# Seven half-depth products in place of eight for two chunks of a feed-forward layer's first product (TensorE, GpSimd)

## The chip, the cores and the metric

The kernel runs on one core of one Trainium2 chip. The metric is the device time of one execution in microseconds (us); the runs are given by their median.

## The reference, cut to what matters

An attention stage is followed by two feed-forward layers. The attention output `x` is taken as 1536 tokens by 512 features.

```python
def _moe_ref(x, w_in, w_out, a, b):        # first layer, d_ff = 2048
    h = x @ w_in
    ...
    return g @ w_out
def _moe2_ref(x, w_in, w_out):             # second layer, d_ff = 2048
    h = x @ w_in
    g = h - np.tanh(h)
    return g @ w_out
```

The change is in `h = x @ w_in` of the second layer: 1536x512 by 512x2048, in fp32.

## The kernel before, in words

Attention takes the first third of the time and is not touched. Each feed-forward layer is cut into three chunks of 512 tokens (`c`) and 16 weight tiles of 128 hidden units (`j`). One *step* `t` is one tile of one chunk; there are 48 steps in each layer, 96 in all (`NT`), and layer, chunk and tile of a step come from `place` (L758).

fp32 precision is had from three matmuls on rounded parts: every operand is kept as `hi` (rounded to fp32r) and `lo` (the rest), and hi*hi, hi*lo and lo*hi are summed in PSUM. So the first product of a step (`pe_g1`, L786) is 4 slices of depth x 3 terms = 12 matmuls of 128x512 into one of four PSUM banks `h_ps`, and the second (`pe_g2`, L811) is 4 blocks x 3 terms = 12 matmuls into the four banks `acc`, where the 16 tiles of a chunk are summed. TensorE's order is written out by hand (L1287): the first product of step t+4 (SKEW = 4), then the second of step t.

In the second layer a step asks of the other engines: ScalarE takes the tanh out of PSUM into `mag` (L880), VectorE subtracts it from `h_ps` into `pol` (L1019), ScalarE rounds that to `g_hi` (L857), which first waits until the second product of three steps earlier has freed one of the three buffers, and VectorE makes `g_lo` (L1025). In chunk 0, each step also splits one `w_in` and one `w_out` tile into hi and lo (L887 and L894 on ScalarE, L1033 and L1041 on VectorE); all 32 weight tiles stay in SBUF for the chunks 1 and 2. The layer's input of each chunk is copied out of `acc` (L911, `x2_raw`), rounded (L916) and its rest made (L1049), with the raw value and the rest in the same memory. The output leaves `acc` through VectorE's copies (L1060) and one store per 128 tokens on SP's queue (L1270 on). SP's queue loads the second layer's weights as the tiles of the first come free (L1267 on). GpSimd has no work in the feed-forward layers but for the splitting of 9 late tiles of the first (`pool_split_weights`, L763).

```python
for t in range(NT):                        # TensorE, L1287
    if t + SKEW < NT:
        pe_g1(eng, t + SKEW)
    pe_g2(eng, t)
```

Of the kernel before, what the change touches and what calls it, by code (L numbers as in the profile page):

```python
# [13 lines left out]
P = 128  # L14
# [16 lines left out]
def build(nc, q, k, v, proj, w_in1, w_out1, coef_a, coef_b, w_in2, w_out2,  # L31
# [42 lines left out]
            for names in ADDED_BY.values() for name in names}  # L74
    loads = {name: top.enter_context(nc.semaphore("s_" + name))
             for name in ["ident", "consts", "coefs", "ready", "coef", "proj", "q", "k", "v", "out", "ops0", "ops1",
# [7 lines left out]
                 "x2_raw", "x2_lo", "y", "early_hi", "early_lo", "low", "sum",  # L84
                 "last_norm", "last_hi", "last_lo"]}

# [4 lines left out]
    with top:  # L91
# [28 lines left out]
        g_lo = sb(top, "g_lo", [P, TEMPS, CH], F32R)  # L120

        def weight_slot(ctx, name):
            hi = sb(ctx, name + "_hi", [P, 512], F32R)
# [53 lines left out]
        for kind, j in LATE:  # L177
            (w_in_slot if kind == "in" else w_out_slot)[j] = weight_slot(mlp, f"w{kind}{j}")
        y_sb = [sqr[:, 0, :], sqr[:, 1, :], sqr[:, 2, :], mag[:, 2, :]]
        h_ps = [ps(mlp, f"h_ps{i}", [P, CH]) for i in range(4)]  # L180
        acc = [ps(mlp, f"acc{i}", [P, 512]) for i in range(4)]
# [589 lines left out]
        def pool_split_tiles(eng, numbers):  # L771
            for i in numbers:
# [3 lines left out]
                else:  # L776
                    pool_split_weights(eng, loads[f"w_out{j}"], w_out_slot[j], i)

        def split_in_count(layer, j):
# [31 lines left out]
        def pe_g2(eng, t):  # L811
            layer, c, j = place(t)
            _, w_hi, w_lo = w_out_slot[j]
            hi, lo = g_hi[:, t % TEMPS, :], g_lo[:, t % TEMPS, :]
            if c == 0:
                if layer == 0 and j < POOL_OUT:
                    eng.wait_ge(mlp_sems["early_lo"], POOL_TILES.index(("out", j)) + 1)
                else:
                    eng.wait_ge(mlp_sems["w_out_lo"], split_out_count(layer, j))
            eng.wait_ge(mlp_sems["g_lo"], t + 1)  # L820
            if t == 0:
                eng.wait_ge(sems["pt_lo"], BIAS + 2 * TILES * PAIRS)
                eng.wait_ge(mlp_sems["sum"], GROUPS)
            for i in range(4):
                cs = slice(i * P, (i + 1) * P)
                if j == 0 and t > 0:
                    if layer == 0 or c == 0:
                        eng.wait_ge(mlp_sems["x2_raw"], 4 * (t // J - 1) + i + 1)
                    else:
                        eng.wait_ge(mlp_sems["y"], 4 * (c - 1) + i + 1)  # L830
                if layer == 0:
                    terms = ((w_lo[:, cs], hi), (w_hi[:, cs], hi), (w_hi[:, cs], lo))
                else:
                    terms = ((hi[:, cs], w_lo[:, :]), (hi[:, cs], w_hi[:, :]), (lo[:, cs], w_hi[:, :]))
                for n, (l, r) in enumerate(terms):
                    mm = eng.matmul(acc[i][:, :], l, r if layer else r[:, :], start=j + n == 0,  # L836
                                    stop=j == J - 1 and n == 2)
                if j == J - 1 and i < 3:
                    mm.then_inc(mlp_sems["acc"], 1)
            mm.then_inc(mlp_sems["g2"], 1)  # L840


        def act_inverse_ln(eng, t):
# [4 lines left out]
        def act_inverse_exp(eng, t):  # L848
            eng.wait_ge(mlp_sems["ln"], t + 1)
            eng.activation(mag[:, t % TEMPS, :], mag[:, t % TEMPS, :], ACT.Exp, scale=-1.0  # L850
                           ).then_inc(mlp_sems["r0"], 1)

        def act_g_hi(eng, t):
            eng.wait_ge(mlp_sems["g"], t + 1)
            if t >= TEMPS:
                eng.wait_ge(mlp_sems["g2"], t - TEMPS + 1)
            eng.activation(g_hi[:, t % TEMPS, :], pol[:, t % TEMPS, :], ACT.Copy  # L857
                           ).then_inc(mlp_sems["g_hi"], 1)

        def act_reads(eng, t):  # L860
            b, hp = t % TEMPS, h_ps[t % 4][:, :]
            if place(t)[0] == 0:
                if t == 0:
                    for e in range(2):
                        eng.wait_ge(loads[f"ops{e}"], 128 * PAIRS)
                    eng.wait_ge(sems["lo"], BIAS + 2 * PAIRS)
                eng.wait_ge(mlp_sems["h"], t + 1)
                if t >= TEMPS:
                    eng.wait_ge(mlp_sems["g_lo"], t - TEMPS + 1)
                eng.activation(pol[:, b, :], hp, ACT.Identity, scale=ca[:, 3:4], bias=ca[:, 2:3])  # L870
                if t >= TEMPS:
                    eng.wait_ge(mlp_sems["g"], t - TEMPS + 1)
                eng.activation(mag[:, b, :], hp, ACT.Abs, scale=cb[:, 0:1])
                eng.activation(sqr[:, b, :], hp, ACT.Square).then_inc(mlp_sems["square"], 1)
            else:
                eng.wait_ge(mlp_sems["h"], t + 1)
                eng.wait_ge(mlp_sems["g"], t - 1)
                if t >= NT - J + SKEW:
                    eng.wait_ge(mlp_sems["y"], 4 * (NCH - 1))
                eng.activation(mag[:, t % 2, :], hp, ACT.Tanh).then_inc(mlp_sems["tanh"], 1)  # L880
# [38 lines left out]
        def act_x2(eng, t):  # L919
            c, step = x2_step(t)  # L920
            if 0 <= c < NCH and step == 0:
                act_x2_raw(eng, c)
            if 0 <= c < NCH and 1 <= step <= 4:
                act_x2_hi(eng, c, step - 1)

        def act_step(eng, t, reads=True):
# [14 lines left out]
            else:  # L941
                if t == L:
                    act_inverse_ln(eng, t - 1)
                    act_g_hi(eng, t - 2)
                    act_inverse_exp(eng, t - 1)
                if t < NT:
                    act_reads(eng, t)
                act_g_hi(eng, t - 1)
                act_x2(eng, t)
                if t < NT:  # L950
                    act_split_in(eng, t)
                    act_split_out(eng, t)


# [67 lines left out]
        def dve_g_lo(eng, t):  # L1022
            b = t % TEMPS
            eng.wait_ge(mlp_sems["g_hi"], t + 1)
            eng.tensor_tensor(g_lo[:, b, :], pol[:, b, :], g_hi[:, b, :].bitcast(F32),  # L1025
                              ALU.subtract).then_inc(mlp_sems["g_lo"], 1)
# [17 lines left out]
        def dve_x2(eng, t):  # L1044
            c, step = x2_step(t)
            if 0 <= c < NCH and 1 <= step <= 4:
                i = step - 1
# [4 lines left out]

        def dve_y(eng, c):
            for i in range(4):
                acc_ready(eng, NCH + c, i)
                if c == 0 and i == 0:
                    eng.wait_ge(mlp_sems["g"], TILES_LAYER)
                if c > 0:
                    eng.wait_ge(loads["out"], 64 * c)
                eng.tensor_copy(y_sb[i], acc[i][:, :]).then_inc(mlp_sems["y"], 1)  # L1060

        def dve_step(eng, t):
# [15 lines left out]
            else:  # L1078
                if t == L:
                    dve_g_lo(eng, t - 2)  # L1080
                    dve_inverse_times(eng, t - 1)
                    dve_g_neg(eng, t - 1)
                if t < NT:
                    dve_g_minus(eng, t)
                dve_g_lo(eng, t - 1)
                dve_x2(eng, t)
                if t < NT:
                    dve_split_in(eng, t)
                    dve_split_out(eng, t)
            if t % J == SKEW - 1 and t >= L + J:  # L1090
                dve_y(eng, (t - L) // J - 1)

        with nc.Block() as block:

            @block.sync
            def _(eng):
# [88 lines left out]
                def load_weight(layer, kind, j):  # L1185
# [7 lines left out]
                    else:  # L1193
                        if layer == 1:
# [3 lines left out]
                                      ).then_inc(loads[f"w_out{j}"], 16)  # L1198

                def sync_att(p, turn=True):  # L1200
                    if turn:
# [68 lines left out]
                for c in range(NCH):  # L1270
                    for i in range(4):
                        block = 4 * c + i
                        eng.wait_ge(mlp_sems["y"], block + 1)
                        eng.dma_start(out_d[:, block // T, block % T, :], y_sb[i]
                                      ).then_inc(loads["out"], 16)
                eng.wait_ge(loads["out"], 64 * NCH)

            @block.tensor
            def _(eng):
# [6 lines left out]
                pe_att(eng, PAIRS - 1, prepare=False, turn=False, last=True)  # L1286
                for t in range(NT):  # L1287
                    if t + SKEW < NT:
                        pe_g1(eng, t + SKEW)
                    pe_g2(eng, t)  # L1290

            @block.scalar
            def _(eng):
# [10 lines left out]
                act_att(eng, PAIRS - 1, prepare=False, turn=False, last=True)  # L1304
                for t in range(2, NT + 1):
                    act_step(eng, t)

            @block.vector
            def _(eng):
# [65 lines left out]
```

## Time and profile before

| | |
|---|---|
| median of 3 runs | 766.28 us (766.01 to 767.57) |
| the profiled execution, its own time | 768.19 us |
| its span, first to last instruction | 766.4 us |
| TensorE busy | 753.4 us, 98% of the span, 3840 matmuls |
| VectorE, ScalarE, GpSimd busy | 536.4, 478.0, 160.6 us |
| mean granted TensorE clock | 0.996 |

The span starts at the first instruction. A matmul's end is modelled, and matmuls are pipelined, so neighbours overlap in the rows; the distance of two starts tells what one costs. PE is TensorE's matmul side, PEld its weight loads, DVE VectorE, ACT ScalarE, POOL GpSimd, and a q behind a name (SPq) the engine's queue of instructions.

### The profile page before, as it was taken

The numbers are of one execution on the slowest core, as the hardware profiler recorded it, in microseconds if no ns is written. First come the engines' busy times: TensorE is split into PE (matmuls) and PEld (weight loads), VectorE is DVE, ScalarE is ACT, GpSimd is POOL, SyncE is SP. The second block draws the span as 40 slices with busy tenths as digits, with TensorE's granted clock in tenths as the row PEclk, the third lists the DMA queues.
The fourth block names the chain that finished last, engine by engine and source line by source line (L and its number), as shares of the span: only waits on it lengthen the run. The fifth ranks groups of instructions, "written<-read, shape, count | busy, mean of one in ns | idle before, by whom it ended". The sixth has DMA issues, their size and how long they took to land.

```text
span 766.4 us, 11961 instructions
## 1 busy us (share of the span) xinstructions
PE 753.4 (98%) x3840; PEld 644.6 (84%) x3840; DVE 536.4 (70%) x854; ACT 478.0 (62%) x938; POOL 160.6 (21%) x137
## 2 busy tenths in 40 slices
PE   5999999999999999999999999999999999999998
PEld 3999999999998788778888888888888888888886
DVE  4888888888997999999988898955542322233222
ACT  4989889888897778788767776755432222222221
POOL 5774574565579000000000000000000000000000
PEclk8999999999999999999999999999999999999999
DMA  7579778777655500000000123230000100001001
GB/s 196 128 173 211 171 171 199 177 178 180 163 128 154 183 1 1 0 1 1 0 1 15 55 86 107 88 91 1 0 1 1 56 0 1 0 1 56 0 1 56
DMA packets 65243, 58.11 MB, mean 76 GB/s; under 512 B 31792, under 2 KB 50480, under 8 KB 65200
## 3 DMA queue, kind: packets, MB, share of 16 engines
q1 hardware_dynamic: 63488, 57.09, 29.6%
q10 hardware_dynamic: 1712, 0.46, 0.3%
q8 instruction: 25, 0.41, 0.2%
q14 instruction: 18, 0.15, 0.1%
HBM read 29.57 MB, written 3.19 MB: 43 GB/s over the span
## 4 chain that ended last, share of the span: by engine, by line
PE 84%; DVE 12%; issue 2%; ACT 1%; ACTq 0%
PE acc L836 28%; PE h_ps L807 27%; PE slot L256 9%; PE turn_ps L382 8%; PE pv_ps L340 4%; PE pv_ps L342 4%; DVE pol L1001 2%; DVE sqr L980 2%; DVE pol L1012 2%; DVE pol L987 1%; DVE pol L993 1%; PE aux_ps L269 1%; DVE sqr L1004 1%; DVE g_lo L1025 1%; DVE wout_lo L1041 1%
## 5 line engine op out<-in xcount | busy, mean ns | idle before, releaser
L807 PE MATMUL h_ps<-x_hi,win_lo 128*128 128x512 f32 x384 | 149.7, 390 | 0.0
L807 PE MATMUL h_ps<-x_lo,win_hi 128*128 128x512 f32 x384 | 149.4, 389 | 0.0
L807 PE MATMUL h_ps<-x_hi,win_hi 128*128 128x512 f32 x384 | 149.4, 389 | 0.0
L857 ACT ACTIVATE g_hi<-pol 128x512 fp32r<-128x512 f32 x96 | 60.8, 634 | 126.0 <-PE acc L836 100.4
L1025 DVE TENSOR_TENSOR g_lo<-pol,g_hi 128x512 fp32r<-128x512 f32 x96 | 66.0, 687 | 97.9 <-ACT g_hi L857 97.7
L623 DVE TENSOR_TENSOR pt_lo<-turn_ps,pt_hi 128x384 fp32r<-128x384 f32 x192 | 97.8, 551 | 20.8 <-ACT pt_hi L530 20.0
L530 ACT ACTIVATE pt_hi<-turn_ps 128x384 fp32r<-128x384 f32 x192 | 85.0, 493 | 21.4 <-PE turn_ps L382 20.8
L581 DVE TENSOR_REDUCE row_min<-slot 128x1 f32<-128x768 f32 x96 | 90.8, 946 | 3.2 <-PE slot L256 2.8
L462 ACT ACTIVATE E<-slot,row_min 128x768 f32<-128x768 f32 x96 | 87.5, 911 | 1.9 <-issue 1.3
L807 PEld LDWEIGHTS h_ps<-x_lo,win_hi 128*128 128x128 f32 x384 | 72.2, 188 | 15.1
L807 PEld LDWEIGHTS h_ps<-x_hi,win_hi 128*128 128x128 f32 x384 | 72.1, 188 | 14.9
L807 PEld LDWEIGHTS h_ps<-x_hi,win_lo 128*128 128x128 f32 x384 | 72.1, 188 | 14.7
L382 PE MATMUL turn_ps<-ident,E 128*128 128x128 f32 x576 | 80.8, 275 | 0.0
L1019 DVE TENSOR_TENSOR pol<-h_ps,mag 128x512 f32<-128x512 f32 x48 | 33.2, 691 | 67.7 <-ACT mag L880 67.2
L880 ACT ACTIVATE mag<-h_ps 128x512 f32<-128x512 f32 x48 | 28.7, 598 | 78.4 <-PE h_ps L807 75.2
L836 PE MATMUL acc<-g_hi,wout_lo 128*128 128x512 f32 x192 | 75.0, 391 | 1.6 <-ACT x_raw L911 0.7
L836 PE MATMUL acc<-g_lo,wout_hi 128*128 128x512 f32 x192 | 74.7, 389 | 0.0
L836 PE MATMUL acc<-g_hi,wout_hi 128*128 128x512 f32 x192 | 74.7, 389 | 0.0
L836 PE MATMUL acc<-wout_lo,g_hi 128*128 128x512 f32 x192 | 74.7, 389 | 0.0
L836 PE MATMUL acc<-wout_hi,g_hi 128*128 128x512 f32 x192 | 74.7, 389 | 0.0
L836 PE MATMUL acc<-wout_hi,g_lo 128*128 128x512 f32 x192 | 74.7, 389 | 0.0
L382 PEld LDWEIGHTS turn_ps<-ident,E 128*128 128x128 f32 x576 | 68.1, 141 | 6.1 <-DVE pt_lo L623 0.6
(119 smaller groups left out, 1383.9 us busy)
## 6 DMA issues: line engine op xcount, KB each, us to landing
win_raw<-in_moe_w_in SPq DMA_DIRECT2D x32, 256.0 KB, 3.3
wout_raw<-in_moe_w_out SPq DMA_DIRECT2D x32, 256.0 KB, 3.0
q_nat<-in_q SPq DMA_DIRECT2D x16, 192.0 KB, 3.3
v_nat<-in_v SPq DMA_DIRECT2D x8, 384.0 KB, 3.3
k_nat<-in_k SPq DMA_DIRECT2D x14, 192.0 KB, 3.5
qA<-q_hi SPq DMA_DIRECT2D x14, 192.0 KB, 2.5
qB<-q_hi SPq DMA_DIRECT2D x14, 192.0 KB, 2.9
qB<-q_lo SPq DMA_DIRECT2D x14, 192.0 KB, 3.2
```

Source lines behind the costliest of these rows:

```text
L256: mm = eng.matmul(slot[m % 2][:, h, 0:HALF], ops[e][0][:, i * P:(i + 1) * P], ops[e][1][:, h * HALF:(h + 1) * HALF], start=first, stop=not ...
L340: eng.matmul(pv_ps[:, 0:HALF], vv, pt_hi[:, c % 2, kt, :], start=kt == 0, stop=False)
L382: mm = eng.transpose(turn_ps[h][:, c3 * P:(c3 + 1) * P], E[:, n % RING, kt * P:(kt + 1) * P], ident[:, :])
L462: eng.activation(halves(E[:, m % RING, :]), slot[m % 2][:, :, 0:HALF], ACT.Exp, bias=row_min[:, m % RING:m % RING + 1], scale=-1.0, accum_ ...
L530: eng.activation(pt_hi[:, c % 2, k0:k0 + T // 2, i * P:(i + 1) * P], turn_ps[h][:, 0:HALF].rearrange("r (k n) -> r k n", n=P), ACT.Copy).t ...
L581: eng.tensor_reduce(row_min[:, m % RING:m % RING + 1], slot[m % 2][:, :, 0:HALF], AX.XY, ALU.min).then_inc(sems["rowmin"], 1)
L623: eng.tensor_tensor(pt_lo[dst], turn_ps[h][:, 0:HALF].rearrange("r (k n) -> r k n", n=P), pt_hi[dst].bitcast(F32), ALU.subtract).then_inc( ...
L807: mm = eng.matmul(h_ps[t % 4][:, :], w[:, ws], columns(x, kt, c), start=kt + n == 0, stop=kt == KT - 1 and n == 2)
L836: mm = eng.matmul(acc[i][:, :], l, r if layer else r[:, :], start=j + n == 0, stop=j == J - 1 and n == 2)
L857: eng.activation(g_hi[:, t % TEMPS, :], pol[:, t % TEMPS, :], ACT.Copy).then_inc(mlp_sems["g_hi"], 1)
L1019: eng.tensor_tensor(pol[:, t % TEMPS, :], h_ps[t % 4][:, :], mag[:, t % 2, :], ALU.subtract).then_inc(mlp_sems["g"], 1)
L1025: eng.tensor_tensor(g_lo[:, b, :], pol[:, b, :], g_hi[:, b, :].bitcast(F32), ALU.subtract).then_inc(mlp_sems["g_lo"], 1)
```

## The change

For the chunks 1 and 2 of the second layer, the input and two weight tiles are taken as 2x2 blocks (two halves of depth by two chunks, and two halves of depth by two tiles). The four results come from seven half-depth products of 6 matmuls each, where before there were four full ones of 12 (eight halves). It is Winograd's form of Strassen's scheme. TensorE's work of the steps 0 to 59 stays as it is; `PLAIN` = 64 is the first step of chunk 1.

- The sums of input blocks (T1 to T4) are made once by VectorE in the steps 53 to 56 (`dve_sums`, 8 instructions), then the seven blocks are split in the steps 56 to 62 (14 roundings on ScalarE, 14 differences on VectorE). The 16 roundings and differences of chunks 1 and 2's own input (8 on each engine) fall away. T2, T3 and T4 take `w_out` slots 0 to 5.
- The sums of weight blocks (S1 to S4) are made once for each pair of tiles by GpSimd (`pool_s`): 10 sums of 128x256, then two roundings and two differences of 128x512. There are two buffers for them: `w_out` slots 6 and 7, and columns of chunk 0's input.
- TensorE (`pe_pair`) does for each of the 8 pairs the seven products, with second products in between: in pair 0 those of steps 60 to 63, one behind each of the products 0 to 3, in each later pair two of chunk 1, one behind product 3 and one behind product 6. Both second products of chunk 1 of pair 7 and the 16 of chunk 2 follow at the end.
- For each pair VectorE does 7 additions out of PSUM, 4 differences h - tanh(h) and 2 `g_lo` (`dve_pair`); ScalarE one copy out of PSUM, 4 tanh and 2 `g_hi` (`act_pair`). The values g of chunk 2 are kept in the `w_in` slots of the even tiles, which the pair has used.
- The eight overwritten `w_out` tiles are loaded and split again (`AGAIN`), one per pair (two in pair 1), into columns of chunk 0's input and the `w_in` slots of the odd tiles. The output of chunk 0 is copied in pair 0, three blocks in the middle, and the fourth, whose buffer waits for the first three stores, at its end.

```diff
+        PER_PAIR = 7
+        NPAIR = J // 2
+        BLOCKS = ["X11", "X21", "T2", "T3", "T1", "T4", "X22"]
+        WEIGHTS = ["W11", "W12", "S2", "S3", "S1", "W22", "S4"]
+        TAKEN = ["p1", "c11", "u2", "u3", "u4", "c21", "c12"]
+        RAW_STEP = PLAIN - 11
+        SPLIT_STEP = PLAIN - 8
+        S_OPS = 14
+        u_sum, u_more = pol[:, 2, :], mag[:, 2, :]
+        AGAIN = [0, 1, 7, 6, 5, 4, 3, 2]
+        AGAIN_STEP = [0, 1, 1, 2, 3, 4, 5, 6]
+        def bank(u, k):
+            return h_ps[(PER_PAIR * u + k) % 4][:, :]
+        def pe_product(eng, u, k):
+            if u == 0 and k < 4:
+                eng.wait_ge(mlp_sems["g"], PLAIN - 3 + k)
+            else:
+                eng.wait_ge(mlp_sems[TAKEN[(k - 4) % PER_PAIR]], u + (k >= 4))
+            if u == 0:
+                eng.wait_ge(mlp_sems["t_lo"], 2 * (k + 1))
+            if k in (2, 3):
+                eng.wait_ge(mlp_sems["s_ops"], S_OPS * u + 8 + 2 * k)
+            for kt in range(2):
+                w_hi, w_lo = w_block(u, WEIGHTS[k], kt)
+                _, b_hi, b_lo = x_block(BLOCKS[k], kt)
+                for n, (w, x) in enumerate(((w_lo, b_hi), (w_hi, b_hi), (w_hi, b_lo))):
+                    mm = eng.matmul(bank(u, k), w, x, start=kt + n == 0, stop=kt + n == 3)
+            mm.then_inc(mlp_sems["prod"], 1)
+        def pe_pair(eng, u):
+            t = PLAIN + 2 * (u - 1)
+            for k in range(PER_PAIR):
+                pe_product(eng, u, k)
+                if u == 0 and k < 4:
+                    pe_g2(eng, PLAIN - 4 + k)
+                if u > 0 and k == 3:
+                    pe_g2(eng, t)
+            if u > 0:
+                pe_g2(eng, t + 1)
...
+        def pool_s(eng, u):
...
+            eng.wait_ge(mlp_sems["w_in_lo"], split_in_count(1, pair_tile(u) + 1))
+            if u == 0:
+                eng.wait_ge(mlp_sems["g2"], TILES_LAYER + S_SLOT + 2)
+            elif u == 1:
+                eng.wait_ge(mlp_sems["h"], PLAIN)
+            else:
+                eng.wait_ge(mlp_sems["prod"], PER_PAIR * (u - 1))
+            sum_(a[:, one], h2[:, one].bitcast(F32), h2[:, two], ALU.add)
+            sum_(b[:, one], h1[:, one].bitcast(F32), h2[:, one], ALU.subtract)
+            sum_(a[:, one], a[:, one], l2[:, one], ALU.add, 1)
+            sum_(b[:, one], b[:, one], l1[:, one], ALU.add, 2)
+            sum_(a[:, one], a[:, one], l2[:, two], ALU.add, 3)
+            sum_(b[:, one], b[:, one], l2[:, one], ALU.subtract, 4)
+            sum_(a[:, two], a[:, one], h1[:, one], ALU.subtract, 5)
+            sum_(a[:, two], a[:, two], l1[:, one], ALU.subtract, 7)
+            sum_(b[:, two], h1[:, two].bitcast(F32), a[:, two], ALU.subtract, 8)
+            sum_(b[:, two], b[:, two], l1[:, two], ALU.add, 9)
+            for i, (raw, hi, lo) in enumerate(((a, a_hi, a_lo), (b, b_hi, b_lo))):
+                eng.wait_ge(mlp_sems["s_ops"], n + 10)
+                eng.tensor_copy(hi, raw).then_inc(mlp_sems["s_ops"], 1)
+                eng.wait_ge(mlp_sems["s_ops"], n + 11 + 2 * i)
+                eng.tensor_tensor(lo, raw, hi.bitcast(F32), ALU.subtract).then_inc(mlp_sems["s_ops"], 1)
...
+        def dve_pair(eng, u):
+            t, n = PLAIN + 2 * u, PER_PAIR * u
...
+            def add(k, out, other, signal):
+                eng.wait_ge(mlp_sems["prod"], n + k + 1)
+                eng.tensor_tensor(out, bank(u, k), other, ALU.add).then_inc(mlp_sems[signal], 1)
+            def minus_tanh(k, out, h, signal):
+                eng.wait_ge(mlp_sems["tanh2"], 4 * u + k + 1)
+                eng.tensor_tensor(out, h, mag[:, k % 2, :], ALU.subtract).then_inc(mlp_sems[signal], 1)
...
+            add(1, first, u_sum, "c11")
+            add(2, u_sum, u_sum, "u2")
+            add(3, second, u_sum, "u3")
+            add(4, u_more, second, "c22")
+            add(4, u_sum, u_sum, "u4")
+            if u == 0:
+                dve_y(eng, 0, range(3))
+            minus_tanh(0, first, first, "g")
+            add(5, second, second, "c21")
+            minus_tanh(1, kept_g(tile + 1), u_more, "kept")
+            dve_g_lo(eng, t)
+            add(6, u_sum, u_sum, "c12")
+            minus_tanh(2, second, second, "g")
+            minus_tanh(3, kept_g(tile), u_sum, "kept")
+            dve_g_lo(eng, t + 1)
+            if u == 0:
+                dve_y(eng, 0, range(3, 4))
...
-                for t in range(NT):
-                    if t + SKEW < NT:
-                        pe_g1(eng, t + SKEW)
+                for t in range(PLAIN - SKEW):
+                    pe_g1(eng, t + SKEW)
+                    pe_g2(eng, t)
+                for u in range(NPAIR):
+                    pe_pair(eng, u)
+                for t in range(NT - J - 2, NT):
                     pe_g2(eng, t)
```

## Rows read from the trace of the kernel before

**Rows 1.** The page: span, busy time of each engine, 40 slices of the span.
```profile
span 766.4 us, 11961 instructions
PE 753.4 (98%) x3840; PEld 644.6 (84%) x3840; DVE 536.4 (70%) x854; ACT 478.0 (62%) x938; POOL 160.6 (21%) x137
...
PEclk8999999999999999999999999999999999999999
```

**Rows 2.** The chain that ended last, in order of time: start us, us, what.
```profile
344.30 2.72 PE h_ps L807 x12
347.02 2.72 PE acc L836 x12
...
749.58 13.61 PE acc L836 x60
```

**Rows 3.** Windows, second layer: us, then busy (xcount) of PE, PEld, DVE, ACT, POOL.
```profile
680.00:760.00 80.00, 80.00 (x354) 66.26 (x354) 21.98 (x33) 17.25 (x28) 0.00 (x0) 1.00 0.04 14
```

**Rows 4.** Groups of DVE and ACT from 330 us on: busy us, mean ns | idle.
```profile
L1025 DVE TENSOR_TENSOR g_lo<-pol,g_hi 128x512 fp32r<-128x512 f32 x81 | 55.7, 688 | 97.9 <-ACT g_hi L857 97.7
L1019 DVE TENSOR_TENSOR pol<-h_ps,mag 128x512 f32<-128x512 f32 x48 | 33.2, 691 | 67.7 <-ACT mag L880 67.2
...
L1060 DVE COPY sqr<-acc 128x512 f32<-128x512 f32 x9 | 5.8, 685 | 4.7 <-PE acc L836 4.7
L857 ACT ACTIVATE g_hi<-pol 128x512 fp32r<-128x512 f32 x81 | 51.3, 634 | 112.3 <-PE acc L836 100.4 <-DVE pol L1012 10.9 <-DVE pol L1019 1.0
L880 ACT ACTIVATE mag<-h_ps 128x512 f32<-128x512 f32 x48 | 28.7, 598 | 78.4 <-PE h_ps L807 75.2 <-DVE mag L1060 3.2
```

**Rows 5.** Groups of POOL over the whole span, shapes apart.
```profile
L687 POOL TENSOR_TENSOR v_hl<-v_nat,v_hl 128x384 fp32r<-128x384 f32 x16 | 16.2, 1010 | 1.3
...
L653 POOL TENSOR_TENSOR k_lo<-k_t,k_hi 128x768 fp32r<-128x768 f32 x7 | 12.9, 1840 | 0.6
...
L768 POOL TENSOR_TENSOR wout_lo<-wout_raw,wout_hi 128x512 fp32r<-128x512 f32 x6 | 7.7, 1287 | 0.5
```

**Rows 6.** Timeline of POOL, 240 to 249 us: start us, us, what.
```profile
240.07 0.61 POOL L766 CAST wout_hi<-wout_raw 128x512 fp32r<-128x512 f32 x1
...
243.93 1.08 POOL L766 CAST wout_hi<-wout_raw 128x512 fp32r<-128x512 f32 x1
245.09 1.29 POOL L768 TENSOR_TENSOR wout_lo<-wout_raw,wout_hi 128x512 fp32r<-128x512 f32 x1
246.32 1.08 POOL L766 CAST win_hi<-win_raw 128x512 fp32r<-128x512 f32 x1
247.48 1.62 POOL L768 TENSOR_TENSOR win_lo<-win_raw,win_hi 128x512 fp32r<-128x512 f32 x1
```

**Rows 7.** Timeline of DVE over the same stretch.
```profile
243.48 1.06 DVE L980 SCALAR_TENSOR_TENSOR sqr<-sqr,cb_abs,mag 128x512 f32<-128x512 f32 x1
...
245.18 0.75 DVE L993 SCALAR_TENSOR_TENSOR pol<-pol,ca,h_ps 128x512 f32<-128x512 f32 x1
245.84 1.09 DVE L1001 SCALAR_TENSOR_TENSOR pol<-pol,ca,mag 128x512 f32<-128x512 f32 x1
246.86 1.09 DVE L1004 SCALAR_TENSOR_TENSOR sqr<-sqr,q_one,mag 128x512 f32<-128x512 f32 x1
247.99 1.67 DVE L1012 SCALAR_TENSOR_TENSOR pol<-sqr,pol 128x512 f32<-128x512 f32 x1
```

**Rows 8.** Timeline around 536 us, in the second layer's chunk 0.
```profile
535.46 0.69 DVE L1025 TENSOR_TENSOR g_lo<-pol,g_hi 128x512 fp32r<-128x512 f32 x1 [2.12 <-ACT g_hi L857]
...
536.07 0.68 DVE L1049 TENSOR_TENSOR x_lo<-x_raw,x_hi 128x512 fp32r<-128x512 f32 x1
...
537.03 0.39 PE L807 MATMUL h_ps<-x_lo,win_hi 128*128 128x512 f32 x1
...
537.45 0.60 ACT L880 ACTIVATE mag<-h_ps 128x512 f32<-128x512 f32 x1 [0.46 <-PE h_ps L807]
```

**Rows 9.** DMA issues: xcount, KB each, median us to landing.
```profile
wout_raw<-in_moe_w_out SPq DMA_DIRECT2D x32, 256.0 KB, 3.0
...
out<-sqr SPq DMA_DIRECT2D x9, 256.0 KB, 2.1
```

More of the change, by code:

```diff
@@ L84, in build @@
                  "x2_raw", "x2_lo", "y", "early_hi", "early_lo", "low", "sum",
-                 "last_norm", "last_hi", "last_lo"]}
+                 "last_norm", "last_hi", "last_lo",
+                 "t_raw", "t_hi", "t_lo", "s_ops", "prod", "p1", "u2", "u3", "u4", "c11", "c22", "c21", "c12",
+                 "tanh2", "kept"]}
     def begin(eng, who):
@@ L812, in pe_g2 @@
             layer, c, j = place(t)
-            _, w_hi, w_lo = w_out_slot[j]
+            if t >= PLAIN:
+                j = kept_tile(t)
+            _, w_hi, w_lo = again_slot[j] if t >= PLAIN and j in again_slot else w_out_slot[j]
+            first, last = t % J == 0, t % J == J - 1
             hi, lo = g_hi[:, t % TEMPS, :], g_lo[:, t % TEMPS, :]
@@ L825, in pe_g2 @@
                 cs = slice(i * P, (i + 1) * P)
-                if j == 0 and t > 0:
+                if first and t > 0:
                     if layer == 0 or c == 0:
@@ L835, in pe_g2 @@
                 for n, (l, r) in enumerate(terms):
-                    mm = eng.matmul(acc[i][:, :], l, r if layer else r[:, :], start=j + n == 0,
-                                    stop=j == J - 1 and n == 2)
-                if j == J - 1 and i < 3:
+                    mm = eng.matmul(acc[i][:, :], l, r if layer else r[:, :], start=first and n == 0,
+                                    stop=last and n == 2)
+                if last and i < 3:
                     mm.then_inc(mlp_sems["acc"], 1)
@@ new lines, in s_buffer, with w_block @@
+        def s_buffer(u):
+            if u % 2 == 0:
+                return [[part[:, :] for part in w_out_slot[S_SLOT + i]] for i in range(2)]
+            return [[columns(part, i, 0) for part in (x2_raw, x_hi, x_lo)] for i in range(2)]
+        def w_block(u, name, kt):
+            half = lambda t, i: t[:, (2 * i + kt) * P:(2 * i + kt + 1) * P]
+            if name[0] == "S":
+                n = int(name[1]) - 1
+                _, hi, lo = s_buffer(u)[n // 2]
+                return half(hi, n % 2), half(lo, n % 2)
+            _, hi, lo = w_in_slot[pair_tile(u) + (name[1] == "2")]
+            return half(hi, name[2] == "2"), half(lo, name[2] == "2")
@@ L1045, in dve_x2 @@
             c, step = x2_step(t)
-            if 0 <= c < NCH and 1 <= step <= 4:
+            if c == 0 and 1 <= step <= 4:
                 i = step - 1
@@ L1051, in dve_x2, with y_buffer, dve_y @@
                                   ).then_inc(mlp_sems["x2_lo"], 1)
-        def dve_y(eng, c):
-            for i in range(4):
+        def y_buffer(c, i):
+            return y_sb[0 if c == 0 and i == 3 else i]
+        def dve_y(eng, c, blocks=range(4)):
+            for i in blocks:
                 acc_ready(eng, NCH + c, i)
@@ L1198, in load_weight, with store_y @@
                                       ).then_inc(loads[f"w_out{j}"], 16)
+                def store_y(c):
+                    for i in range(4):
+                        block = 4 * c + i
+                        eng.wait_ge(mlp_sems["y"], block + 1)
+                        eng.dma_start(out_d[:, block // T, block % T, :], y_buffer(c, i)
+                                      ).then_inc(loads["out"], 16)
                 def sync_att(p, turn=True):
@@ L1269, in _ @@
                     load_weight(1, "out", j)
[L1270 to L1275, printed above, removed]
+                eng.wait_ge(mlp_sems["h"], PLAIN)
+                for r, j in enumerate(AGAIN):
+                    if r == 2:
+                        store_y(0)
+                    if r >= 2:
+                        eng.wait_ge(mlp_sems["prod"], PER_PAIR * (r - 2) + 6)
+                    eng.dma_start(again_slot[j][0][:, :], w_out2[j * P:(j + 1) * P, :]
+                                  ).then_inc(loads[f"w_out{j}"], 16)
+                store_y(1)
+                store_y(2)
                 eng.wait_ge(loads["out"], 64 * NCH)
```

162 lines of the change are left out of this document (147 added, 15 removed).

## The prediction

> **What bounds the kernel now.** I read the page first. TensorE is busy for 98% of the span, and its granted clock is nine tenths or more in all slices after the first [rows 1]: the time is the number of matmuls times what one costs, wherever nothing holds TensorE up. The chain of waits says how far that is true of the second layer: first and second products take turns, 2.72 us for 12 matmuls each, up to a last piece of 60 in 13.61 us [rows 2]. There is not one wait in between, and one matmul costs 13.61 / 60 = 0.2268 us. A window of that layer shows what the others do meanwhile: of 80 us TensorE is busy 80, VectorE 22, ScalarE 17, GpSimd nothing [rows 3]. Their waits are on TensorE (100.4 us of `g_hi` on `acc`, 75.2 us of tanh on `h_ps`) [rows 4]. So a matmul less is worth 0.2268 us, until another engine is late.
>
> **What is removed.** Chunks 1 and 2 had 32 first products of 12 matmuls, 384. Now they have 8 pairs x 7 products x 6 = 336. The 48 fewer are worth 48 x 0.2268 = **10.88 us**, all of it on the path. TensorE's new timetable, if nobody is late (a product 1.36 us, a second product 2.72): pair 0 takes 7 x 1.36 + 4 x 2.72 = 20.4 us, later pairs 7 x 1.36 + 2 x 2.72 = 14.96 us, and then come 18 second products as dense as now. Would more and shorter products cost something at their borders? Where h_ps gives way to acc, rows show no gap [rows 2], so I take 0; the other end is a rival below.
>
> **VectorE in a pair.** It has 7 additions from PSUM, 4 differences, 2 `g_lo` and mostly one `lo` of a reloaded tile: 14 instructions of 0.69 us, the time of its present forms [rows 4]. Started behind each other they come every 0.61 us (535.46 to 536.07) [rows 8]. That is 8.5 to 9.7 us of 14.96. ScalarE has 8 of 0.60 to 0.63 us [rows 4], 5 us. Both fit, and the waits are loose: a product's bank must be free four products later. Counted from the start of a later pair, product 4 ends at 9.52 us, products 5 and 6 at 10.88 and 12.24. The last addition (c12) can start at about 13.4 and end at 14.1, and product 3 of the next pair, at 19.04, waits for it; `g_lo` of the pair's first tile ends near 13.5 and is wanted at 20.4 (14.96 in pair 7, at the end). So these waits cost 0, covered by 1.4 us or more.
>
> **GpSimd, the new work.** The trace has no sum of 128x256, so I bound it. A two-input instruction takes 1.01 us at 384 columns, 1.29 at 512, 1.84 at 768 [rows 5]: between the first two 0.28 us per 128 columns. One step down gives 0.73 us at 256, which I take, being the line of the nearest rows; half of the 512 form (0.64) and the 384 form (1.01) are the ends. A rounding and a difference at 512 take 1.93 us together (four such instructions from 240.07 to 243.93) [rows 6]. One pair: 10 x 0.73 + 2 x 1.93 = 11.2 us (10.3 to 14.0), on an engine otherwise idle.
>
> But it does not run alone. While GpSimd works, VectorE's instructions with both inputs in SBUF take 1.06, 1.09, 1.09 and 1.67 us, and those with one input in PSUM 0.75 as ever [rows 7]; GpSimd's own roundings take 1.08 instead of 0.61, and its last difference 1.62 instead of 1.29 [rows 6]. They take turns. GpSimd loses 0.47, 0.47 and 0.33 us to the three instructions that it waits for: 0.43 each. A pair holds 7 such on VectorE (4 differences, 2 `g_lo`, 1 reloaded `lo`), while the 7 additions read PSUM. GpSimd's pair is then 11.2 + 7 x 0.43 = **14.2 us** (10.3 to 17.0) against 14.96. By the Trainium skill, "SBUF — State Buffer", section "Who interferes with whom", the two share a read interface when VectorE has two SBUF inputs, and the second to come blocks until the first has ended. By that rule, whole durations add up: about 11.2 + 7 x 0.69 = 16.0 us; the rows agree on which instructions are hit, with 0.43 us for each.
>
> What may GpSimd take? Sums u are wanted at products 2 and 3 of pair u and, from u = 2, may start when pair u - 2 has done its seven products. Six sets (2 to 7) lie between the end of pair 0 (20.4) and product 3 of pair 7 (20.4 + 6 x 14.96 + 4.08 = 114.2): 15.6 us each. So 14.2 costs 0, and an excess counts six times. Set 0 starts once the last `w_in` tile is split, in VectorE's step 59, about 20 us ahead of pair 0, and is wanted at 8 us; set 1 may start 2.7 us ahead of pair 0 and is wanted at 23. Both are covered by 10 us.
>
> **VectorE before pair 0.** Steps 53 to 62 gain 8 + 14 instructions and lose 4 of chunk 2; the other 4 lost are in the first layer. A step has 4 to 6 of them in 5.44 us, up to 4.1 us, or some 6.6 with GpSimd beside it in steps 60 to 62. The sum T4 in step 56 waits for the second product of step 53, about 3 us, and the next difference h - tanh(h) is queued behind it. TensorE wants that one 4 steps later, over 15 us. Cost 0; the cover is these four banks.
>
> **From pair 0 to pair 1.** This is the one tight place. VectorE meets three output copies of 0.69 us [rows 4] after product 4. Its results can be used 0.42 us after the last matmul's start (537.03 to 537.45) [rows 8], so 0.2 after the timetable. Product 4 ends at 17.68: c22 starts at 17.88; then u4, three copies, a difference, c21, a difference, `g_lo` come every 0.61 us, and c12 starts at 23.3 and ends at 24.0. Product 3 of pair 1 wants it at 24.48. But set 2 on GpSimd began at 20.4, and three of those nine have two SBUF inputs: +0.3, +0.3, +0.45, by what is left of the GpSimd instruction they meet. So c12 ends at 25.0 and TensorE waits **0.6 us** (0 to 2, with each hit as in [rows 7]: up to 0.98). The fourth output block is ready near 28.4, when its accumulation is due; its three stores need 2.1 us [rows 9], and were issued by 22. The 8 reloads land in 3.0 us [rows 9], one per 15 us, and are split at the end of the pair after the one that frees the slot: 0. They stand on SP's queue ahead of the stores of chunks 1 and 2, which come later anyway. The end (last accumulation, copies, stores) is as before: 0.
>
> **Sum.** -10.88 + 0.6 = -10.3 us. The profiled execution has 768.19 us, span 766.4 and 1.8 around it; it would give 757.9. It stands 1.9 above the median of 766.28, for which I say **756.0 us**. Bounds: 755.0 with no stall and 0.4 of luck between runs.
>
> **Rivals.**
> 1. *GpSimd becomes the bound.* If each hit costs GpSimd a whole VectorE instruction, 0.69 us [rows 4] in place of 0.43, a set takes 11.2 + 7 x 0.69 = 16.0 us, 0.4 above the 15.6 allowed: 6 x 0.4 = 2.4 us, **758.4**. With the upper end (17.0) it is 6 x 1.4 = 8.4, 764.4. For it: GpSimd is 95% loaded by my own sum. Against: a hit cost 0.33 to 0.47 us. 0.15. (The rule of the Trainium skill's page above would come out here.)
> 2. *VectorE becomes the bound.* If each of the 7 hits costs 0.98 us (1.67 less 0.69), a pair takes 14 x 0.61 + 6.9 = 15.4 us, 0.4 over, in seven pairs 3.1 us: **759.1**. Against: only one hit of four was so long, beside a difference of 512 columns; here ten of fourteen GpSimd instructions are half as long. 0.10.
> 3. *Short sums are no shorter, and it gets slower.* If GpSimd's cost is by instruction, 256 columns take 1.29 us. A set takes 10 x 1.29 + 3.86 + 3.0 = 19.8 us, 4.2 over: 6 x 4.2 = 25 us lost, 10.9 won, **780**. It decides against the change from 15.6 + 10.9 / 6 = 17.4 us per set, a sum of 1.05 us. Against: 384, 512 and 768 columns lie on a line. 0.06.
> 4. *It does not pay at all.* If every short product costs 0.2 us at its border, 56 of them give 11.2 us back: **766.6**. Nothing in rows 2 speaks for it. 0.03.
>
> **Chances.** My forecast 0.66, the rivals 0.15, 0.10, 0.06 and 0.03. Faster by over 0.2% (1.5 us, about what a measurement of this kernel can tell from no change) are the forecast and the first two: 0.91; same 0.03; slower 0.06. The range of 8 in 10 runs from 755.0 over the forecast and its 2 us of stall to the rivals 1 and 2 and part of the upper end of a set: 760.5.
>
> **What would show it.** PE: 3792 matmuls, still 0.227 us apart in the pairs. GpSimd: 80 sums near 0.73 us, some of 1.1, a set in 14 to 15 us, busy for some 100 us after the last plain step. TensorE's waits: 0.6 us at product 3 of pair 1 on VectorE's c12, none on `s_ops`. A recurring wait at product 2 or 3 on GpSimd means rival 1 or 3; waits on VectorE's additions in each pair, rival 2; gaps with nobody late, rival 4. I am wrong if the median lies above 760.5 or TensorE has more than 2 us of waits in the pairs.

## The result, and the profile after

The changed kernel takes **757.83 us** (median of 5 runs, 756.29 to 759.45), the kernel before, beside it, 766.01 (765.84 to 767.57). The ratio is 0.9877, with a 95% interval of 0.9860 to 0.9895. I had said 756.0, within 755.0 and 760.5. The profiled execution took 758.12 us; I had said 757.9 for it. Its span went from 766.4 to 756.2 us, 10.2 us less; I had said 10.3.

The page of the changed kernel answers to [rows 1]. I cut section 2 to the lines of the two engines that changed most and of the clock.

```profile
span 756.2 us, 12132 instructions
PE 742.6 (98%) x3792; PEld 635.3 (84%) x3792; DVE 606.6 (80%) x932; ACT 489.7 (65%) x960; POOL 272.8 (36%) x249
...
DVE  4888988888997999999988888975696598885622
...
POOL 5775574574579100000000000000048499993000
PEclk8999999999999999999999999999999999999999
```

TensorE has the 48 matmuls fewer and is as busy as ever. VectorE has 70 us more of busy time and GpSimd 112 us, all of it behind 540 us (63 and 105 us of it behind 567 us, in the last quarter), where four slices of GpSimd show nine tenths. None of this has lengthened the time: what counts is whether TensorE waits, and the chain of waits, which answers to [rows 2], shows one place where it did (start us, us, what; 578.19 is the first product of pair 0).

```profile
578.19 1.36 PE h_ps L976 x6
579.55 2.72 PE acc L886 x12
...
594.51 1.38 PE h_ps L976 x6
...
602.37 0.61 DVE pol L1325
602.98 0.04 issue
603.02 1.66 PE h_ps L976 x6
604.68 2.80 PE acc L886 x12
607.49 4.11 PE h_ps L976 x18
611.60 2.72 PE acc L886 x12
614.32 5.44 PE h_ps L976 x24
...
697.28 4.08 PE h_ps L976 x18
701.36 51.69 PE acc L886 x228
```

From pair 2 on the pieces are the timetable of the prediction to a hundredth: four products in 5.44 us, 2.72, three in 4.08, 2.72. The chain leaves TensorE once, for VectorE's addition c12 (L1325), and comes back at 603.02 with product 3 of pair 1. All waits of TensorE from 576 us to the end are in three rows of the table of waits (us in total, times, longest):

```profile
PEld h_ps L976 <- DVE pol L1325: 0.8, 1, 0.8
PE h_ps L976 <- DVE pol L1325: 0.4, 1, 0.4
PEld acc L886 <- DVE sqr L1259: 0.2, 1, 0.2
```

The first two are the same stop seen at the weight load and at the matmul; the third is the output copy of the fourth block. No row names GpSimd.

For comparing kernels I use a distance inside one trace that leaves out the attention stage. It runs from the start of the first second product of chunk 1 of the first feed-forward layer (the only such piece of 3.00 us, at 341.30 us in the kernel before) to the end of the last piece of second products. Before it is 749.58 + 13.61 - 341.30 = **421.89 us**, after 701.36 + 51.69 - 341.27 = **411.78 us**: 10.11 us less. 48 matmuls at 0.2268 us are 10.88 [rows 2], so 0.77 us is what was lost.

### The profile page after: what moved, and what is told of

The parts are those of the page before. It is cut to its first block, busy times and chain, and to the rows that moved or that the text cites. A ratio compares the mean times of both kernels' runs of the same rounds, so it can differ in the third digit from the quotient of the medians.

```text
span 756.2 us, 12132 instructions
## 1 busy us (share of the span) xinstructions
PE 742.6 (98%) x3792; PEld 635.3 (84%) x3792; DVE 606.6 (80%) x932; ACT 489.7 (65%) x960; POOL 272.8 (36%) x249
## 4 chain that ended last, share of the span: by engine, by line
PE 83%; DVE 12%; issue 2%; ACT 1%; ACTq 0%; DVEq 0%
PE acc L886 29%; PE h_ps L852 16%; PE h_ps L976 9%; PE slot L265 9%; PE turn_ps L391 8%; PE pv_ps L349 4%; PE pv_ps L351 4%; DVE pol L1195 2%; DVE sqr L1174 2%; DVE pol L1206 1%; DVE pol L1181 1%; DVE pol L1187 1%; PE aux_ps L278 1%; DVE sqr L1198 1%; DVE g_lo L1219 1%
## 5 line engine op out<-in xcount | busy, mean ns | idle before, releaser
L852 PE MATMUL h_ps<-x_hi,win_lo 128*128 128x512 f32 x256 | 99.9, 390 | 0.0
L852 PE MATMUL h_ps<-x_lo,win_hi 128*128 128x512 f32 x256 | 99.6, 389 | 0.0
L852 PE MATMUL h_ps<-x_hi,win_hi 128*128 128x512 f32 x256 | 99.6, 389 | 0.0
L1219 DVE TENSOR_TENSOR g_lo<-pol,g_hi 128x512 fp32r<-128x512 f32 x80 | 65.7, 821 | 20.2 <-ACT g_hi L1015 19.8
L351 PE MATMUL pv_ps<-pt_lo,v_hl 128*128 128x384 f32 x192 | 64.6, 337 | 0.0
L349 PE MATMUL pv_ps<-pt_hi,v_hl 128*128 128x384 f32 x192 | 64.5, 336 | 0.0
L1028 ACT ACTIVATE pol<-h_ps,ca 128x512 f32<-128x512 f32 x48 | 37.2, 776 | 40.9 <-PE h_ps L852 38.2
L265 PE MATMUL slot<-kA,qA 128*128 128x384 f32 x192 | 59.7, 392 | 2.1 <-ACT kA L443 1.1
L852 PEld LDWEIGHTS h_ps<-x_lo,win_hi 128*128 128x128 f32 x256 | 48.0, 188 | 10.0
L852 PEld LDWEIGHTS h_ps<-x_hi,win_lo 128*128 128x128 f32 x256 | 48.1, 188 | 9.9
L852 PEld LDWEIGHTS h_ps<-x_hi,win_hi 128*128 128x128 f32 x256 | 48.0, 188 | 9.8
```

The costliest lines, as they stand in the source:

```text
L265: mm = eng.matmul(slot[m % 2][:, h, 0:HALF], ops[e][0][:, i * P:(i + 1) * P], ops[e][1][:, h * HALF:(h + 1) * HALF], start=first, stop=not ...
L349: eng.matmul(pv_ps[:, 0:HALF], vv, pt_hi[:, c % 2, kt, :], start=kt == 0, stop=False)
L351: mm = eng.matmul(pv_ps[:, 0:HALF], vv, pt_lo[:, c % 2, kt, :], start=False, stop=kt == T - 1)
L852: mm = eng.matmul(h_ps[t % 4][:, :], w[:, ws], columns(x, kt, c), start=kt + n == 0, stop=kt == KT - 1 and n == 2)
L1219: eng.tensor_tensor(g_lo[:, b, :], g_made(t), g_hi[:, b, :].bitcast(F32), ALU.subtract).then_inc(mlp_sems["g_lo"], 1)
```

## The experiments

All changes are to the changed kernel, and each has 4 to 12 timed executions, with the kernel before beside it. A median carries the noise of the whole execution, 2 to 3 us; the distance just defined does not.

### The same kernel again

`same` and, in a later series, `same2` alter nothing.

> The changed kernel once more, nothing altered in its work. Theory (48 matmuls fewer, less one wait at the border of pairs 0 and 1): span 756.2 us again within its spread (754.4 to 757.5 in five runs), PE waits in the pairs 0.7 us, distance from the first product of pair 0 to the last second product 174.9 us. If the spread of three us comes out of the pairs (VectorE and GpSimd meeting differently each time), this distance differs from 174.9 by as much as the span does; if it comes from the first third, the distance stays and the start of pair 0 moves.

> The changed kernel once more beside the last one. The stretch from the 3.00 us piece at 340 us to the last second product is 411.7 to 411.8 us whatever the time of the execution; the time itself lies where the first third puts it, 755.8 to 759.5 us, near 756 where the first matmuls run at the full clock and near 758 where they don't.

`same` took 755.96 us (755.77 to 757.82; ratio 0.9853, 0.9834 to 0.9872), `same2` 756.96 (755.77 to 758.77; ratio 0.9876, 0.9855 to 0.9898). The distance is 411.74 and 411.77 us in them, to 0.04 us that of the first trace. So the pairs do not vary between these traces; what varies lies ahead of that mark. The windows of the first series' changed kernel and of `same` (us, then PE busy, its matmuls, the granted clock, DMA share and GB/s) show where:

```profile
15.00:20.00 5.00, 4.07 (x16) 0.50 0.63 204
20.00:25.00 5.00, 4.94 (x36) 0.87 0.29 65
```

```profile
15.00:20.00 5.00, 3.48 (x24) 1.00 0.55 173
20.00:25.00 5.00, 4.88 (x37) 1.00 0.56 127
```

In the first trace TensorE is granted half its clock, 1.2 of 2.4 GHz, between 15 and 20 us: four matmuls of scores take 1.62 us where they take 0.93 in `same`. A matmul that starts at 20.84 us in `same` (the 61st of the trace) starts at 22.79 in the first trace, and the 3.00 us piece at 341.27, against 339.31: 1.96 us, the whole difference of the two spans (756.2 and 754.3). The trace of the kernel before has the slower beginning as well (0.50, 341.30), and so have `twosets` and `latecopy` below, and by the times of its matmuls `sums4`.

### One product twice

```diff
-            for kt in range(2):
+            for kt in ((0, 1, 0, 1) if k == 5 else range(2)):
```

> Product 5 of each pair is computed twice over (6 matmuls more in each of 8 pairs, 3840 in all as before the change), everything else stays. Theory (the gain is the number of matmuls times 0.2268 us): 10.9 us more than the changed kernel, less up to 0.7 us where the added matmuls in pair 0 give VectorE time: 10.2 to 10.9 us more, as slow as the kernel before. Rival (short products cost something at their borders): the time lies above that of the kernel before by what the borders cost, over 1 us.

`twice` took 767.56 us (766.21 to 769.09) beside 768.13 for the kernel before, ratio 1.0001 (0.9987 to 1.0014). Its distance is 709.93 + 51.69 - 339.73 = 421.89 us, to the hundredth that of the kernel before, with the same 3840 matmuls and no wait of TensorE left. That is 10.11 us more than the changed kernel; I had expected 10.2 to 10.9, having put the stall at 0.7 at most. The 48 products that are still short cost nothing at their borders: rival 4 is out, and 10.11 us is 10.88 less a stall of 0.77.

### GpSimd with more to do

Each set's first sum is made once (`sums1`), twice (`sums2`) or four times more (`sums4`); every repeat waits for the one before, since it writes the same place. The counts of the semaphore are moved to suit.

`MORE` is 1, 2 or 4.

```diff
-            sum_(a[:, one], h2[:, one].bitcast(F32), h2[:, two], ALU.add)
+            for i in range(MORE):
+                sum_(a[:, one], h2[:, one].bitcast(F32), h2[:, two], ALU.add, i - MORE if i else 0)
+            n += MORE
+            sum_(a[:, one], h2[:, one].bitcast(F32), h2[:, two], ALU.add, 0.0)
...
-        S_OPS = 14
+        MORE = 1
+        S_OPS = 14 + MORE
```

> Each GpSimd set has its first sum once more (0.81 us with the wait for the one before). Theory (sets 2 to 7 run back to back, the last is ready 6.0 us ahead of its use at product 3 of pair 7, so six times the added time less 6.0 us is lost): 6 x 0.81 = 4.9 us, all inside the slack: no more than 0.3 us change. Rival (GpSimd already bounds the pairs): 4 to 6 us more.

> The first sum of each set twice more (1.62 us). Theory: 6 x 1.62 - 6.0 = 3.7 us more than the changed kernel, in waits of PE on the sums in pairs 5 to 7 only (1.5 us each at most). Rival (a full pair is the limit, 14.96 us, whatever the slack): 8 x 1.3 = 10 us more.

> The first sum of each set four times more (3.24 us). Theory: 6 x 3.24 - 6.0 = 13.4 us more than the changed kernel, slower than the kernel before by some 3 to 5 us; a set takes 17.9 us (14.6 before). Rival (VectorE then meets GpSimd less often as the pairs stretch): 1 to 3 us less than that.

| kernel | median us (range) | ratio to before (95%) | distance us | more than after |
|---|---|---|---|---|
| `sums1` | 757.03 (756.32 to 758.39) | 0.9874 (0.9855 to 0.9893) | 411.75 | 0.0 |
| `sums2` | 759.80 (759.15 to 762.35) | 0.9913 (0.9894 to 0.9932) | 415.39 | 3.6 |
| `sums4` | 770.65 (768.71 to 772.43) | 1.0044 (1.0025 to 1.0063) | 424.38 | 12.6 |

I expected 0, 3.7 and 13.4. The rule of the prediction, six sets between the end of pair 0 and product 3 of pair 7, with everything within the slack free and every excess counted six times, holds on both sides of its limit: the six sets took 93.0 us in `sums1`, 15.5 each, and 97.6 in `sums2`, 16.3 each. In `sums4` they took 106.7, where the 88.3 of the changed kernel and 6 x 3.24 would give 107.7: the loss is 0.8 us under my sum, at the edge of what the rival had (1 to 3). The rival's reason does not hold, though: 50 of VectorE's instructions with two SBUF inputs start during the six sets of `sums4`, against 45 in the changed kernel. What made the sets 1.0 us shorter than the sum is open. `sums4` is the slower case of rival 3 made on purpose: 2.5 us more than the kernel before by the distance. I was wrong about where `sums2` waits. I had said pairs 5 to 7. Its chain goes over to GpSimd's last difference already in pair 3, at 632 us:

```profile
630.30 1.62 POOL x_lo L825
631.91 0.14 issue
632.05 1.62 PE h_ps L980 x6
...
646.02 1.62 POOL wout_lo L825
647.63 0.14 issue
647.77 1.62 PE h_ps L980 x6
```

The sets 2 and 3 are longer than the later ones (15.5 and 15.0 us in the changed kernel, then 14.6), because VectorE comes late out of pair 0 and meets GpSimd more often: 10 of its instructions with two SBUF inputs start during set 2, 8 during set 3, 7 during each of the sets 4 to 6. So the slack is smallest early.

### GpSimd with almost nothing to do

GpSimd makes only the sets 0 and 1. The sums of weight blocks of the pairs 2 to 7 are left out, and these pairs use the first two sets' again.

```diff
             if k in (2, 3):
-                eng.wait_ge(mlp_sems["s_ops"], S_OPS * u + 8 + 2 * k)
+                eng.wait_ge(mlp_sems["s_ops"], S_OPS * min(u, 1) + 8 + 2 * k)
...
-                for u in range(NPAIR):
+                for u in range(2):
                     pool_s(eng, u)
```

> GpSimd makes only the sets of pairs 0 and 1; the pairs 2 to 7 use these again, so their sums of weight blocks are left out. Theory (GpSimd costs TensorE nothing but the wait at product 3 of pair 1): 0.4 to 0.7 us less than the changed kernel; VectorE's differences and g_lo, now 0.74 to 1.21 us on the mean, go back to 0.69, and 8 pairs of it get 3 us shorter each without TensorE being any faster. Rival (sharing costs time in every pair): over 2 us less.

`twosets` took 757.48 us (755.68 to 758.04, ratio 0.9870, 0.9850 to 0.9891), its distance is 700.68 + 51.69 - 341.36 = 411.01 us, 0.77 less than the changed kernel, a little more than the 0.4 to 0.7 that I had expected: exactly the 10.88 us of the matmuls, and no wait of TensorE from 576 us on. (The beginning of the profiled execution, which is also the median one, was of the slower kind, which hides this in the median.) So all that GpSimd costs TensorE in the changed kernel is the stop round pair 1. What it costs VectorE can be read from the groups of VectorE. First the changed kernel from 598.5 to 690 us, while GpSimd works (busy us, mean ns | idle):

```profile
L1325 DVE TENSOR_TENSOR pol<-h_ps,pol 128x512 f32<-128x512 f32 x38 | 25.9, 683 | 0.5
L1219 DVE TENSOR_TENSOR g_lo<-pol,g_hi 128x512 fp32r<-128x512 f32 x13 | 18.1, 1394 | 0.0
L1329 DVE TENSOR_TENSOR pol<-pol,mag 128x512 f32<-128x512 f32 x14 | 13.1, 933 | 0.0
L1362 DVE TENSOR_TENSOR win_lo<-win_raw,win_hi 128x512 fp32r<-128x512 f32 x5 | 6.1, 1222 | 0.0
```

Then `twosets` from 596 us on:

```profile
L1219 DVE TENSOR_TENSOR g_lo<-pol,g_hi 128x512 fp32r<-128x512 f32 x16 | 10.9, 682 | 0.0
L1329 DVE TENSOR_TENSOR pol<-pol,mag 128x512 f32<-128x512 f32 x16 | 10.9, 679 | 0.0
```

The additions out of PSUM (L1325) take 683 ns beside GpSimd and 686 without it. The instructions with both inputs in SBUF take 0.25 to 0.71 us more in the groups shown; the difference of u_more (`win_g`) takes only 0.07 more (750 ns against 679). Over all 48 of them in that stretch it is 0.39 us each.

### The stop at pair 1: three ways round it

`gate` holds GpSimd's set 2 back:

```diff
                 eng.wait_ge(mlp_sems["prod"], PER_PAIR * (u - 1))
+                if u == 2:
+                    eng.wait_ge(mlp_sems["c12"], 1)
```

> GpSimd's set 2 of sums starts only after pair 0's addition c12 instead of at the end of product 6. Theory (GpSimd's beginning there delays VectorE by 1.0 to 1.3 us): with nothing beside it, VectorE's c12 ends 1 us earlier (near 602.0 in place of 602.97) and the wait at product 3 of pair 1 is gone, while set 7 ends up to 4 us later (near 690 in place of 687), still ahead of its use at 693: 0.3 to 0.6 us less in all. Rival (the copies alone make the wait): the wait of 0.36 us stays.

`gate` took 755.95 us (755.56 to 757.19, ratio 0.9852, 0.9834 to 0.9871), distance 411.45: 0.33 us less, at the low end. The stop at product 3 of pair 1 is gone, as the theory has it, so GpSimd's start was needed for it (c12 ends at 600.23 here; this trace runs 1.84 us ahead, so that is 602.07 for 602.97), but a new one stands in pair 2, where the set that was held back is now late. Its chain:

```profile
599.62 0.61 DVE pol L1327
600.23 0.02 issue
600.26 0.04 POOLq L809
600.30 0.09 issue
600.39 6.63 POOL wout_raw L799 x7
...
614.19 1.62 POOL wout_lo L824
615.81 0.14 issue
615.95 1.62 PE h_ps L978 x6
```

I had looked only at set 7's slack (4 us later, 6 to spare). From the end of pair 0 to product 3 of pair 2 there are 14.96 + 4.08 = 19.0 us. Set 2 takes 15.4 of them and here began at 600.39, 3.5 us later than it would have (598.74 less those 1.84 us): nothing is left.

`latecopy` moves the three output copies behind c12:

```diff
-            if u == 0:
-                dve_y(eng, 0, range(3))
             minus_tanh(0, first, first, "g")
...
             add(6, u_sum, u_sum, "c12")
+            if u == 0:
+                dve_y(eng, 0, range(3))
```

> The three copies of chunk 0's output in pair 0 come after the addition c12 instead of ahead of the first difference. Theory (c12 is late by the three copies, 1.8 us, and then by GpSimd): c12 ends 1.8 us earlier, product 3 of pair 1 waits for nothing; 0.4 us less than the changed kernel, and 0.1 to 0.3 us of waits for the fourth output block stay. Rival (TensorE waits for something else there): the 0.36 us wait at product 3 stays.

`latecopy` took 757.93 us (756.33 to 758.11, ratio 0.9867, 0.9845 to 0.9889), distance 411.66: 0.12 less, where I had expected 0.4. The wait at product 3 is gone, and the wait for the fourth output block has grown, because that copy starts when VectorE has done the same work in all, at 605.79 as in the changed kernel:

```profile
605.79 0.69 DVE sqr L1259
606.48 0.04 issue
606.52 0.96 PE acc L886 x3
```

The late thing is VectorE's queue, whatever its order. So `actcopy` takes the three copies out of it and gives them to ScalarE, which has nothing to do there:

```diff
             act_tanh(eng, 0, pol[:, 0, :])
+            if u == 0:
+                for i in range(3):
+                    acc_ready(eng, NCH, i)
+                    eng.activation(y_buffer(0, i), acc[i][:, :], ACT.Copy).then_inc(mlp_sems["y"], 1)
             eng.wait_ge(mlp_sems["c22"], u + 1)
...
             add(4, u_sum, u_sum, "u4")
-            if u == 0:
-                dve_y(eng, 0, range(3))
             minus_tanh(0, first, first, "g")
```

> The first three copies of chunk 0's output in pair 0 are made by ScalarE (behind its first tanh, while it waits for c22) instead of by VectorE. From the four traces of the first series the layer-2 end lies 0.75 us later than matmuls alone would give, all of it VectorE's lateness round the border of pairs 0 and 1. Theory (VectorE's queue there is the whole stall): with 1.87 us taken out of that queue c12 ends near 601.1 us for 602.97, the fourth block is copied early enough, and PE has no wait in the pairs: the stretch from the first second product of chunk 1 of the first layer (the 3.00 us piece at 341 us) to the last second product is 411.0 us, 0.7 less than the changed kernel's 411.8. Rival (ScalarE's copies delay its g_hi and tanh, which are next): waits of PE on g_lo or c12 appear, and the stretch stays at 411.5 or more.

`actcopy` took 755.47 us (754.76 to 757.13, ratio 0.9858, 0.9836 to 0.9880), distance 698.49 + 51.69 - 339.17 = 411.01 us, 0.77 less than the changed kernel and the full 10.88 us below the kernel before. TensorE has no wait in the pairs. VectorE's queue in its trace:

```profile
593.88 0.69 DVE L1329 TENSOR_TENSOR mag<-h_ps,pol 128x512 f32<-128x512 f32 x1 [3.36 <-PE h_ps L976]
594.49 0.68 DVE L1329 TENSOR_TENSOR pol<-h_ps,pol 128x512 f32<-128x512 f32 x1
595.09 0.68 DVE L1333 TENSOR_TENSOR pol<-pol,mag 128x512 f32<-128x512 f32 x1
...
596.89 1.23 DVE L1223 TENSOR_TENSOR g_lo<-pol,g_hi 128x512 fp32r<-128x512 f32 x1
598.04 0.68 DVE L1329 TENSOR_TENSOR pol<-h_ps,pol 128x512 f32<-128x512 f32 x1
```

c12 ends 4.84 us after c22 begins (593.88 to 598.72); in the changed kernel it was 6.99 (595.98 to 602.97). It is the best version here. Its medians lie within the noise of `same` and `same2`; that it is 0.77 us faster than the changed kernel rests on the distance in the traces.

## Why the prediction was right

**The gain.** 48 matmuls at 0.2268 us, 10.88 us: measured to the hundredth, by `twosets` and `actcopy` (421.89 - 411.01) and from the other side by `twice`.

**The stop from pair 0 to pair 1.** I said 0.6 us (0 to 2) at product 3 of pair 1, on c12; it was 0.77 us in all. By the timetable product 3 is due at 578.19 + 20.4 + 4.08 = 602.67 and done at 604.03; it was done at 604.68, 0.65 late. The other 0.12 is the second product behind it, which took 2.80 us for 2.72, and 0.03 after that: the fourth output block, which I had called ready just when due. I had three of nine instructions hit, c12 ending at 25.0 us after the pairs' start; it ended at 602.97 - 578.19 = 24.8. Without GpSimd, in `twosets`, it ended at 23.9, where I had 24.0. Two were hit in fact, by 0.36 (a difference, 1.04 us) and 0.54 (`g_lo`, 1.23 us); one difference of u_more was not hit at all (0.68), since it started just as a GpSimd instruction ended. So the hits came to 0.9 us for my 1.05, and c12 was only 0.3 late. The rest of the 0.65 is a term that I did not have: a product behind a stop takes longer, 1.66 us here for 1.36, and 1.62 at the stops in `gate` and `sums2`. That the stop came out within 0.2 us of my 0.6 is in part luck. `gate` showed that GpSimd's start is needed for the wait at c12, `latecopy` and `actcopy` that the copies are.

**GpSimd.** The short sum was 0.73 us by the line through 384, 512 and 768 columns; it is 0.74 when nothing is beside it. I said 14.2 us per set and 0.43 per hit. The starts of the sets 4 to 7 in the timeline are 14.6 us apart, two of them shown here:

```profile
643.85 2.39 POOL L799 TENSOR_TENSOR x_raw<-win_hi 128x256 f32<-128x256 f32 x2
646.20 4.18 POOL L799 TENSOR_TENSOR x_raw<-x_raw,win_lo 128x256 f32<-128x256 f32 x4
650.33 0.75 POOL L799 TENSOR_TENSOR x_raw<-x_raw,win_hi 128x256 f32<-128x256 f32 x1
...
658.45 2.39 POOL L799 TENSOR_TENSOR wout_raw<-win_hi 128x256 f32<-128x256 f32 x2
```

So a set is (14.6 - 11.3) / 7 = 0.47 us per hit, 11.3 being 10 x 0.74 + 2 x 1.93. In each of the sets 4 to 6 seven of GpSimd's 14 instructions are longer than alone, in the sets 2 and 3 nine and eight: 11.3 + 9 x 0.47 = 15.5 and 11.3 + 8 x 0.47 = 15.1, and they took 15.5 and 15.0. The limit of 15.6 was right, as `sums1` and `sums2` show from both sides, and rival 1 (16.0 us) did not come. The Trainium skill, "SBUF — State Buffer", section "Who interferes with whom", names the instructions that are hit, and the trace agrees: L1329, L1219 and L1362 are, L1325 is not. Its rule that the second to come blocks until the first has ended fits the rows too (see the last section), but whole durations do not add up, which would have made a set 16.0 us long: the second comes when part of the first has already run. The set measured 14.6.

**VectorE.** Its hits cost it up to 1.1 us (a `g_lo` of 1.78), more than the 0.3 to 0.45 I had used and than the 0.98 of rival 2, but 0.39 on the mean. A window of just one set, 643.80 to 658.40, has it busy 11.66 of 14.60 us, so it was not the bound; rival 2 did not come.

**The median.** Here I was 1.8 us low, within the range, though the profiled execution came out to 0.2 us. I had carried over that the profiled execution of the kernel before stood 1.9 us above its median. Such a distance is chance: the two kinds of beginning alone make 2 us of it, and they do not explain all of the spread (the execution of 759.45 us had a mean clock of 1.000; what made it long is open). In the later series the same kernel gave medians of 755.96 and 756.96, 0.0 and 1.0 us above my number, and the kernel before 768.13, 766.58 and 766.50.

## What to carry to other kernels

When one engine is busy all the time and nothing waits in its chain, the worth of an edit is the number of its instructions times their distance, here to the hundredth; all the work of predicting lies in asking each other engine for its first late result. Do that per buffer and per deadline: the slack at the last use says nothing about the slack at the first, as `gate` and `sums2` showed. A copy that any engine could make belongs on the one that is idle at that moment, not on the one whose queue has the next deadline behind it.

## What the runs showed of the hardware

Sharing between VectorE and GpSimd is one of order, not of bandwidth, and a hit has a price that can be computed. The changed kernel at 656 us:

```profile
656.69 1.79 POOL L822 TENSOR_TENSOR x_lo<-x_raw,x_hi 128x512 fp32r<-128x512 f32 x1
657.26 1.77 DVE L1219 TENSOR_TENSOR g_lo<-pol,g_hi 128x512 fp32r<-128x512 f32 x1
```

VectorE's `g_lo` begins when GpSimd's difference has 1.23 us to go, and takes 1.77 us: those 1.23 and 0.54 more. Alone it takes 0.68. For all 48 of VectorE's instructions with two SBUF inputs between 598.5 and 690 us the same sum holds within 0.02 us: the rest of the GpSimd instruction in which it began plus 0.55 us, and 0.68 where that rest was 0.12 us or less or there was none (0.50 us left gave 1.04, 0.68 gave 1.22, 0.99 gave 1.54). GpSimd pays in the same way for the VectorE instruction in which it begins: mostly 1.18 to 1.25 us for a sum of 0.74. So the second waits for the rest of the first, less 0.13 to 0.15 us of its own start. It cost GpSimd 0.47 us per hit and VectorE 0.39 us on the mean, up to 1.1.

The granted clock fell to 0.50 (1.2 GHz) between 15 and 20 us in four of the twelve traces (the kernel before, the changed kernel, `twosets`, `latecopy`) and stayed at 1.00 in `same`, `same2`, `gate` and `actcopy`, with the same work of TensorE up to there; the changed kernel is in both groups. `twice`, `sums2` and `sums1` lie between, with 0.83, 0.85 and 0.78. The fixed mark (the 3.00 us piece) stands at 341.27 to 341.38 us in the first group, at 338.93 to 339.43 in the second, at 339.71 to 340.18 between: the clock is worth 2 us of the span. In the two traces shown, TensorE was busy 7.01 and 7.20 of the 10 us before, which does not tell them apart. In the trace of `sums4` the clock is recorded as 1.00 in that window though a pair of matmuls takes 0.84 us there as in the slower kind (0.51 in `same`), so the row of the clock can miss it. What decides between the kinds was not tried.

The clock also fell once in the pairs, in `sums4` right after TensorE's longest stop there (2.2 us idle up to 635.09):

```profile
635.00:640.00 5.00, 4.91 (x14) 3.61 (x15) 0.76 (x2) 0.08 (x1) 4.65 (x6) 0.66 0.00 0
```

Matmuls then started 0.43 us apart for some 3 us, where they start 0.23 apart elsewhere. It cost nothing more in the end: TensorE had to wait for GpSimd's next set (653.84) all the same.
